# Linear attention and two mixing layers: the last tokens' key sums added by GpSimd, and one wait less at the turn of the maxima

## What is computed

```python
def phi(x):
    proj = np.einsum('bhsd,df->bhsf', x, w_phi)
    proj = proj - np.max(np.abs(proj), axis=-1, keepdims=True)
    return np.concatenate([np.exp(proj), np.exp(-proj)], axis=-1)
q_p, k_p = (phi(q), phi(k))
kv = np.einsum('bhsf,bhsd->bhfd', k_p, v)
z = np.sum(k_p, axis=2)
num = np.einsum('bhsf,bhfd->bhsd', q_p, kv)
den = np.einsum('bhsf,bhf->bhs', q_p, z)[..., None] + 1e-06
return (num / den)
```

## Time and profile before

| what | value |
|---|---|
| median of three runs | 1258.35 us |
| the profiled execution's own time | 1257.32 us |
| its span, first to last instruction | 1255.4 us |
| TensorE busy | 1241.4 us, 99% of the span |
| VectorE, ScalarE busy | 856.1 us (68%), 576.5 us (46%) |
| GpSimd busy | 144.2 us (11%) |
| granted TensorE clock | 0.999 of full speed (2.4 GHz) |

### The profile page before, as it was taken

The page is one execution under the profiler, slowest core; times in us unless marked ns, Lnnn a source line. Parts: engine busy times, 40 slices in busy tenths (PEclk is TensorE's granted clock), DMA queues, the critical chain, the costliest instruction groups (busy, mean ns, idle before and its releaser), DMA issues.

```text
span 1255.4 us, 23373 instructions
## 1 busy us (share of the span) xinstructions
PE 1241.4 (99%) x9332; PEld 1091.3 (87%) x9332; DVE 856.1 (68%) x1372; ACT 576.5 (46%) x1049; POOL 144.2 (11%) x137
## 2 busy tenths in 40 slices
PE   8899999999999999999999999999999999999998
PEld 7678898898888888889889888999989899898897
DVE  7889667677676766866767766648566584683863
ACT  4654643635536545464363543455334343352441
POOL 3412111211112111211121111000000000000000
PEclk9999999999999999999999999999999999999999
DMA  5612122221212222222222121421202102012001
GB/s 182 180 32 70 52 61 61 70 60 52 79 50 61 71 60 61 71 52 60 64 66 60 48 64 49 132 70 39 72 8 73 72 1 80 28 45 80 1 34 42
DMA packets 88243, 78.89 MB, mean 63 GB/s; under 512 B 58440, under 2 KB 67016, under 8 KB 87112
## 3 DMA queue, kind: packets, MB, share of 16 engines
q1 hardware_dynamic: 87976, 77.33, 20.4%
q10 hardware_dynamic: 160, 0.07, 0.0%
HBM read 58.21 MB, written 19.01 MB: 62 GB/s over the span
## 4 chain that ended last, share of the span: by engine, by line
PE 93%; DVE 4%; issue 1%; ACT 1%; DMA 0%; POOL 0%; SPq 0%; DVEq 0%; POOLq 0%
PE psm L610 40%; PE ps L610 20%; PE psh L1296 6%; PE psh L1297 6%; PE psh L1295 6%; PE pso L1297 5%; PE pso L1296 5%; PE pso L1295 5%; PE ps L721 1%; DVE q_part L1038 1%; DVE q_turn L1035 1%; DVE mix L1115 0%; DVE k_max L1028 0%; DVE den_first L1087 0%; PE ps L675 0%
## 5 line engine op out<-in xcount | busy, mean ns | idle before, releaser
L610 PE MATMUL psm<-xy_hi,wk_hi 128*128 128x288 f32 x512 | 155.7, 304 | 2.5 <-DVE xy_lo L1134 1.8
L610 PE MATMUL psm<-k_hi,wv_hi 128*128 128x288 f32 x512 | 153.7, 300 | 0.0
L1297 PE MATMUL psh<-xy_hi,win_lo 128*128 128x288 f32 x512 | 151.3, 296 | 0.0
L1295 PE MATMUL psh<-xy_hi,win_hi 128*128 128x288 f32 x512 | 151.3, 296 | 0.0
L1296 PE MATMUL psh<-xy_lo,win_hi 128*128 128x288 f32 x512 | 151.3, 296 | 0.0
L610 PE MATMUL psm<-xy_lo,wk_hi 128*128 128x288 f32 x512 | 151.2, 295 | 0.0
L610 PE MATMUL psm<-k_lo,wv_hi 128*128 128x288 f32 x512 | 151.0, 295 | 0.0
L610 PE MATMUL psm<-k_hi,wv_lo 128*128 128x288 f32 x512 | 150.8, 295 | 0.0
L610 PE MATMUL psm<-xy_hi,wk_lo 128*128 128x288 f32 x512 | 150.8, 294 | 0.0
L598 POOL TENSOR_TENSOR z_pairs<-k_signs 128x512 f32<-128x512 f32 x56 | 74.3, 1327 | 578.5 <-ACT k_signs L876 565.3
L876 ACT ACTIVATE k_signs<-k_signs 128x1152 f32<-128x1152 f32 x32 | 37.2, 1163 | 163.0 <-DVE k_signs L1030 151.6
(11 more groups left out here) (159 smaller groups left out, 2824.9 us busy)
## 6 DMA issues: line engine op xcount, KB each, us to landing
k_in<-in_k SPq DMA_DIRECT2D x32, 320.0 KB, 3.5
v_nat<-in_v SPq DMA_DIRECT2D x32, 320.0 KB, 3.7
q_in<-in_q SPq DMA_DIRECT2D x32, 288.0 KB, 3.1
y_scr<-y SPq DMA_DIRECT2D x64, 144.0 KB, 1.9
y<-y_scr SPq DMA_DIRECT2D x8, 1152.0 KB, 5.7
den<-den_scr SPq DMA_DIRECT2D x60, 144.0 KB, 3.0
out<-rows SPq DMA_DIRECT2D x32, 256.0 KB, 2.1
stage<-in_moe_w_in SPq DMA_DIRECT2D x4, 512.0 KB, 3.7
```

The costliest lines, as they stand in the source:

```text
L610: return nc.tensor.matmul(o, lhsT, rhs, start=first, stop=last, skip_group_check=True)
L1295: nc.tensor.matmul(o, wh, xh, start=first, stop=False, skip_group_check=True)
L1297: return nc.tensor.matmul(o, wl, xh, start=False, stop=last, skip_group_check=True)
```

## The change

Four places. GpSimd adds tile 8, on the 64 partitions of each head, into that head's part of `z_tiles`, in place, after a wait for its own second presum: two instructions a pair, with no wait between them. TensorE waits for `z_added` in place of `z_presummed` and leaves out the products with tile 8. M no longer waits for `k_tail_shifted`. VectorE's part of the last K tile (K, n, 7) is no longer brought out ahead of the tile R 0 but ahead of R 1, that is behind the VectorE steps that lie between them: in batches 1 to 7 behind E and RC of pair 1 (n = 0) and behind M, DV and XK, HK (n = 1); in the last iteration behind XK, HK, LK of the second half and the weight piece W 2 (n = 0), and behind W 4 (n = 1).

```diff
-        if step[0] in ("K", "K+", "R", "V"):
+        if step[0] in ("K", "K+", "R", "V") and step[0::2] != ("R", 0):
             out += tile
             tile = []
...
+        def add_last_tokens(p, a):
+
+            pool.wait_ge(z_presummed, 2 * PAIRS * (a - 1) + 2 * p + 2)
+            for h in range(2):
+                own = slice(D * h, D * h + TAIL)
+                nc.gpsimd.tensor_tensor(z_tiles[own, :, h, :], z_tiles[own, :, h, :], k_signs[own, :, KEYS - 1, :], ALU.add).then_inc(z_added, 1)
+
         for a in range(1, B):
             for p in range(PAIRS):
                 for e in range(2):
                     presum(p, a, e)
+                add_last_tokens(p, a)
...
         def turn_maxima(p, a):
             await_(pe, q_part_ready, PAIRS, a, p + 1)
-            await_(pe, k_tail_shifted, PAIRS, a, p + 1)
...
-            pe.wait_ge(z_presummed, 2 * PAIRS * (a - 1) + 2 * p + 2)
-            for t in (0, TT - 1):
-                for h in range(2):
-                    for e in range(2):
-                        row = 32 * (2 * h + e)
-                        last = mm(sums_turned()[row:row + 1, 2, :], v_nat[:, t, h, D:D + 1],
-                                  k_signs[:, e, KEYS - 1, :] if t else z_tiles[:, e, h, :], t == 0, t == TT - 1)
+            pe.wait_ge(z_added, 2 * PAIRS * (a - 1) + 2 * p + 2)
+            for h in range(2):
+                for e in range(2):
+                    row = 32 * (2 * h + e)
+                    last = mm(sums_turned()[row:row + 1, 2, :], v_nat[:, 0, h, D:D + 1], z_tiles[:, e, h, :], True, True)
             last.then_inc(kv_summed, 1)
```

More of the change, by code:

```diff
@@ L335, in phase_1 @@
     kv_summed, kvz_copied = sem("kv_summed"), sem("kvz_copied")
-    z_paired, z_presummed, kvt_copied, kv_turned, z_copied = (
-        sem("z_paired"), sem("z_presummed"), sem("kvt_copied"), sem("kv_turned"), sem("z_copied"))
+    z_paired, z_presummed, z_added, kvt_copied, kv_turned, z_copied = (
+        sem("z_paired"), sem("z_presummed"), sem("z_added"), sem("kvt_copied"), sem("kv_turned"), sem("z_copied"))
     features, q_exp_ready = sem("features"), sem("q_exp_ready")
```

## The result

The changed kernel takes 1254.37 us (median of 20 runs, 1253.58 to 1258.89) against 1258.40 for the kernel before (20 runs, 1256.37 to 1261.90). The ratio is 0.9972, with a 95% interval of 0.9965 to 0.9980: 2.5 to 4.4 us faster. The profiled execution took 1255.47 us, 1.85 less than that of before, with a span of 1253.7.

The account below looks back on a forecast made before the run. TensorE was taken as the bound in batches 1 to 7. The terms -6.2 - 0.85 + 2.3 + 0.2 = -4.55 gave 1252.8 us, plus 1.0 to the median 1253.8; 8-in-10 range 1250.9 to 1257.0.

Parts of the forecast that it names:

- the likeliest case: Whole kernel: GpSimd keeps its turn over both adds; 1253.8 us, own range 1252.3 to 1255.3, chance 0.42.
- Eight instructions less: TensorE's products with tile 8 in 28 pairs: 0.22 us gained in each, 6.2 us in all.
- M's wait: Opening, batch 0, pair 3: M freed from the shifted tail's wait gains 0.85 us, between 0 and 0.9.
- with L590 0.85 earlier, L1090 is too: Opening: VectorE's L1090 stood still for GpSimd's L590, so both move 0.85 us; 0 if another VectorE input is late next.
- The cover of the two adds: KV: the adds end 1.56 us after the last presum, under TensorE's 20 value products; least spare 0.2 us.
- VectorE slips in: Pairs 1 to 3: VectorE runs between the adds; costs 3.7 us, sum -3.4, 1254.9 us; chance 0.20.
- The maxima come late: Pairs 0 and 3: adds of 0.9 us delay `max_blocks`, TensorE waits 14 times 0.25; 1257.3 us, chance 0.11.
- Pair 0: Batches 2 to 7: the adds hold back L1049 and L1052, PICK 0.06 us late, six times; 0.2 in batch 1.
- Batch 1, pair 1: Late last presum: PICK at 104.2 to 104.9 instead of 103.47; costs 0.75 to 1.4 us, 1.4 taken.
- The last K tile: Its low part made later: 0.2 us lost in the last iteration (0 to 0.4), nothing in batches 1 to 7.
- Slower: VectorE and GpSimd alternate over the adds, each waiting for a VectorE instruction: +6.5 us, 1265 us; chance 0.07.
- The overlap of the two adds: GpSimd works both adds side by side, done 0.8 us after the presum: -6.1 us, 1252.2 us; chance 0.20.

Follow-up runs that it names:

- left_out: Kernel before with VectorE's new order for the last K tile and the tile 8 products removed, nothing in their place: 1251.86 us, ratio 0.9951.
- m_only: Kernel before with only M's wait for the shifted tail removed: 1258.27 us, ratio 1.0000.
- adds_unawaited: left_out plus GpSimd's two adds, written to `z_pairs`, with TensorE not waiting for them: 1254.22 us, ratio 0.9973 against the kernel before.
- m0_first: The change, with VectorE taking the maxima's chain ahead of K tile 3's low part at pair 0: 1256.69 us, ratio 0.9990 against the kernel before.

## Why the prediction was right, and where not

Forecast 1253.8, measured 1254.37, inside the 1252.3 to 1255.3 of the likeliest case. The direction and the gross gain were right; that the number is so near is in part luck, as the terms show.

- **Eight instructions less, -6.2**: right. left_out measured 5.7 in the middle part, 5.9 with the first pair, and 6.4 by the medians.
- **M's wait, -0.85**: nothing was measured, 0 within 1.1 us (m_only, 0.9991 to 1.0009), and the openings with the wait gone (80.7 to 85.8) are no shorter than those with it (80.6 to 85.3). The step that failed is "with L590 0.85 earlier, L1090 is too". L590 was 0.08 earlier and not 0.85, as the whole opening had shifted, and the denominator's transfer, at 55.9, was VectorE's later input. The bound of 0 that I had kept for that case was the value.
- **The cover of the two adds and who goes first**: this is where the forecast took the wrong branch. I held that two GpSimd instructions with no wait between them leave no gap. The second add starts 0.07 us after the first ends, and VectorE's waiting instruction goes in between: adds of 0.93 on average, up to 1.35, in place of 0.74. Two signs that the prediction had named came up: a wait for GpSimd at pair 3, which was to tell of this branch, and adds of over 0.9, which it had called a sign that the forecast is wrong. The price was near what the rival "VectorE slips in" had: at pair 3 the z products were 0.33 late, 0.26 of it as idle time, where 0.25 stood. It met four of seven batches; in the other three `max_blocks` came behind both adds, and PICK was late by 0.14. Pair 1 lost 0.09 to 0.26 where I had 0 to 0.2. In all, the middle part is 3.5 and 2.7 us over left_out in the two executions of the change, where 2.1 stood (2.3 less the 0.2 of batch 1, pair 0, which lies before it). The rival "The maxima come late" had its condition met, adds of 0.9, but not its price: PICK was late by 0.16 at pair 0 and by 0.14 at three pairs 3, not by 0.25 at fourteen.
- **Pair 0**: 0.16 lost at PICK instead of 0.06: L1057 waited for the end of the second add, up to 0.1 later than worked out. As 0.09 of it comes back at the turn and behind it, 0.07 is left (adds_unawaited, an iteration), so the term's size was met, but only because of two gains that it didn't have. In batch 1 it was 0.29 instead of 0.2.
- **Batch 1, pair 1**: PICK at 104.57, inside the 104.2 to 104.9; the pair lost 0.76 and its 0.22, 1.0 where the sum took 1.4.
- **The last K tile**: 0.24 in the last iteration, 0.2 stood. Between batches 1 and 7 nothing, as the cover named held.

The rival's sum was -3.4, which leaves out the 0.2 of the last K tile; with it, and with the M term at 0, it is -2.3. (The sum of the rival "Slower" is off too: its terms make +6.15, not +6.5.) The parts of the two executions of the change give -1.8 (0.19 - 2.20 + 0.24) and -2.65 (0.21 - 3.02 + 0.16), their own times against that of before -1.85 and -2.73, and the lowest run of each kernel -2.8 (1256.37 and 1253.58). The medians give -4.0. So the number 1253.8 came nearer to the median than its terms deserve: the terms erred to the side of the gain, M's by 0.85, the adds' by 0.6 to 1.4 and the eight instructions' by 0.3, and some 1.2 us of the medians' distance is not in the traces' accounts. Whether that is the opening, which moves by some microseconds from execution to execution, stays open; no experiment held it fixed. The overlap of the two adds did not take place, and neither did the alternation that would have made the kernel slower: the longest add, 1.35, stood still for 0.6, and no batch lost more than 0.33 at pair 3.

## What to carry to other kernels

Work moved to a helper engine has to be timed with the neighbour that shares its way to SBUF: look in the trace for two-input instructions of either engine whose durations jump, and count an added instruction once for its own time and once for each neighbour it meets, in both directions. Where two chains, here the adds and the maxima, both end at the same engine, bringing one forward can make the other the late one, so put their ends side by side per pair before changing an order. Where products overlap in strips, count them per strip: taking some off the list saves nothing as long as one strip keeps all of its own. And read a new order in every iteration that it touches: the order of m0_first gained nothing where it was meant to and lost 1.0 us in the last iteration.

## What the runs showed that was not expected

- Two GpSimd instructions with no semaphore between them, on partitions 0 to 63 and 64 to 127, do not overlap and leave 0.07 to 0.08 us between them in all 28 pairs. The memsets of the opening had overlapped by 0.06. The rule cited from the Trainium skill, "GPSIMD Engine Reference", section Instruction dispatch, would have let cores without a share in the first add begin the second; for these instructions the trace does not agree.
- An add over 64 partitions takes as long as one over 128: 0.72 to 0.73 us undisturbed for 256 elements, against 0.74.
- The same program falls into either of two patterns from batch to batch: at pair 3 `max_blocks` sometimes goes between the adds and sometimes behind them, 3.65 or 3.42 us, with no difference in the list. A difference of a few ns goes with it: by the start times of the single instructions, L1057 starts 3 to 5 ns after the first add in the four batches of the change where it takes 0.19, so that `max_blocks` is waiting when the first add ends. It starts 6 or 7 ns after it in the three where it stands still up to the end of that add (0.77), so that `max_blocks` comes up only when the second add has begun. Why the few ns matter, no run here shows.
